# Three small edits to a sequence-block kernel: who issues the first keys' transfer, where a variance row is copied, and how the last product is added and stored

## The reference

```python
# attention, 8 heads of 64: heads 0-3 see the last 32 positions, heads 4-7 every 32nd position
scores = (q @ k.T) / 8; scores = where(mask, scores, -1e9)
x = softmax(scores) @ v                        # heads side by side: 4 x 576 x 512
# gated unit, 512 -> 1024 -> 512
h = gelu(x @ w_in); u, v = h[..., :512], h[..., 512:]
v_n = layer_norm(v) * g_ln
x = x + (u * (w_sg @ v_n + b_sg)) @ w_out      # w_sg mixes the 576 tokens
# norm and feed-forward, 512 -> 2048 -> 512
xn = layer_norm(x) * g_ch                      # over the 512 features
out = x + relu(xn @ w_ch1) @ w_ch2
```

## Time and profile before

| what | value |
|---|---|
| median of 3 runs | 666.21 us (666.0, 666.21, 667.43) |
| profiled execution, its own time | 666.58 us |
| its span | 664.8 us, 14064 instructions |
| PE busy, PE weight loads busy | 655.3 us (99%), 622.8 us (94%) |
| DVE, ACT, POOL busy | 529.1 us (80%), 356.8 us (54%), 245.9 us (37%) |
| chain that ended last | PE 89%, DVE 4%, issue 2%, ACT 2%, POOL 2% |

### The profile page before, as it was taken

How to read it: one execution, slowest core, us unless ns; L and a number is a source line. 1 busy time by engine, 2 the same in 40 slices (tenths; PEclk the granted TensorE clock), 3 DMA queues, 4 the chain that set the end, 5 groups by cost and what they waited for, 6 DMA issues and landing times.

```text
span 664.8 us, 14064 instructions
## 1 busy us (share of the span) xinstructions
PE 655.3 (99%) x5160; PEld 622.8 (94%) x5160; DVE 529.1 (80%) x1162; ACT 356.8 (54%) x897; POOL 245.9 (37%) x258
## 2 busy tenths in 40 slices
PE   8999999999999999999999999999999999999997
PEld 4679998999899998999999999999999999999997
DVE  5967866887679868998876885786999898898883
ACT  6866864488347844434563462345684344444440
POOL 0477240635152438468436447223001412113011
PEclk9999999999999999999999999999999999999999
DMA  8660007000530051128353667869952726517301
GB/s 296 258 241 4 1 3 278 36 1 2 186 146 2 1 176 59 56 69 291 119 171 121 199 241 251 306 216 348 303 171 84 290 72 246 165 58 282 90 19 53
DMA packets 49924, 98.25 MB, mean 148 GB/s; under 512 B 4673, under 2 KB 33217, under 8 KB 47297
## 3 DMA queue, kind: packets, MB, share of 16 engines
q1 hardware_dynamic: 49152, 96.16, 42.2%
q0 software_dynamic: 704, 1.21, 0.8%
HBM read 64.83 MB, written 32.52 MB: 146 GB/s over the span
## 4 chain that ended last, share of the span: by engine, by line
PE 89%; DVE 4%; issue 2%; ACT 2%; POOL 2%; DVEq 0%; POOLq 0%; ACTq 0%
PE pair L1886 17%; PE pair L1888 17%; PE pair L1887 17%; PE pair L1677 9%; PE pair L1679 9%; PE pair L1678 9%; PE pair L1701 3%; PE pair L1734 3%; PE pair L1716 3%; ACT probs L1026 1%; DVE stage L1546 1%; PE pair L1685 1%; DVE res L1406 1%; DVE acc_a L489 1%; PE pair L1797 1%
## 5 line engine op out<-in xcount | busy, mean ns | idle before, releaser
L1886 PE MATMUL pair<-xf_hi,w_hi 128*128 128x288 f32 x896 | 265.6, 296 | 0.2
L1887 PE MATMUL pair<-xf_lo,w_hi 128*128 128x288 f32 x896 | 264.5, 295 | 0.0
L1888 PE MATMUL pair<-xf_hi,w_lo 128*128 128x288 f32 x896 | 263.6, 294 | 0.0
L1888 PEld LDWEIGHTS pair<-xf_hi,w_lo 128*128 128x128 f32 x896 | 168.8, 188 | 0.0
L1886 PEld LDWEIGHTS pair<-xf_hi,w_hi 128*128 128x128 f32 x896 | 167.9, 187 | 0.8 <-ACT rstd L1103 0.7
L1887 PEld LDWEIGHTS pair<-xf_lo,w_hi 128*128 128x128 f32 x896 | 168.2, 188 | 0.0
L1131 ACT ACTIVATE xf_hi<-res 128x576 fp32r<-128x576 f32 x140 | 94.3, 683 | 89.1 <-PE pair L1888 71.9
L1546 DVE TENSOR_TENSOR stage<-pair,stage 128x576 f32<-128x576 f32 x136 | 100.7, 752 | 39.5 <-PE pair L1888 33.3
L567 DVE TENSOR_TENSOR xf_lo<-res,xf_hi 128x576 fp32r<-128x576 f32 x140 | 109.8, 793 | 14.7 <-ACT xf_hi L1131 14.2
L1012 POOL TENSOR_TENSOR xr<-xr,stage 128x576 f32<-128x576 f32 x16 | 32.9, 2058 | 165.7 <-DVE stage L1546 165.6
L1223 ACT ACTIVATE stage<-stage 128x576 f32<-128x576 f32 x64 | 43.6, 683 | 79.8 <-DVE stage L1546 79.7
(11 more groups left out here) (134 smaller groups left out, 1285.0 us busy)
## 6 DMA issues: line engine op xcount, KB each, us to landing
hid_scratch<-stage SPq DMA_DIRECT2D x64, 288.0 KB, 3.5
res<-hid_scratch SPq DMA_DIRECT2D x16, 1152.0 KB, 6.8
w_raw<-w_ff_dram SPq DMA_DIRECT2D x16, 512.0 KB, 4.2
v_sb<-vW_dram SPq DMA_DIRECT2D x16, 384.0 KB, 6.7
xr<-x_scratch SPq DMA_DIRECT2D x16, 288.0 KB, 3.0
out_dram<-xr SPq DMA_DIRECT2D x16, 288.0 KB, 3.3
k_sb<-kT_dram SPq DMA_DIRECT2D x15, 304.0 KB, 6.3
q_sb<-qT_dram SPq DMA_DIRECT2D x15, 288.0 KB, 6.2
```

The costliest lines, as they stand in the source:

```text
L1886: pe.matmul(dst, wh, xh, start=(start and x == 0), stop=False)
L1887: pe.matmul(dst, wh, xl, start=False, stop=False)
L1888: last = pe.matmul(dst, wl, xh, start=False, stop=(stop and x == n - 1))
```

## The change

It has three parts.

First, the first keys' transfer leaves SP's list and becomes the first instruction of ACT's program. On SP the masks' transfer is now second, and everything behind it moves up one place. The warm-up ahead of the first scores has five matmuls and not six.

Second, on ACT, `copy_variance(b - 1, 0)` moves in periods 1 and 2 from the end of t = 0 to just behind the exponentials of step 0.

Third, for the last batch alone, the last product's two halves are handled apart: PE signals `half_ready` when half 0 of its last piece is done, DVE adds half 0 then and half 1 when the product is complete, and SP issues one store of 144 KB for each half in place of one of 288 KB.

```diff
--- before.py
+++ after.py
@@ -77,6 +77,7 @@
 SOLO_WIN_ACT = 2
 WIN_HALVES = (slice(GATE, 2 * GATE), slice(0, GATE))
 EARLY = 4
+NQ_FIRST, NK_FIRST = 2 * QB, 2 * QB + STRIDE
 
 
 FORMS = 7
@@ -351,9 +352,11 @@
         hid_stored = [sem(f"hid_stored{i}") for i in range(4)]
         raw_in = [sem(f"raw_in{i}") for i in range(4)]
         step_ready = sem("step_ready")
+        half_ready, half_added = sem("half_ready"), sem("half_added")
         y_added = sem("y_added")
         waited = sem("waited")
         stored = [sem(f"stored{i}") for i in range(4)]
+        stored_half = sem("stored_half")
 
         block = ctx.enter_context(nc.Block())
 
@@ -632,9 +635,8 @@
                         load_win(0)
                     nq, nk = 0, 0
                     if first and pair == 0:
-                        nq, nk = 2 * QB, 2 * QB + STRIDE
+                        nq, nk = NQ_FIRST, NK_FIRST
                         sp.dma_start(q_sb[:, 0, 0:nq], qT[b, :, 0, 0:nq]).then_inc(q_first, 16)
-                        sp.dma_start(k_sb[:, 0, 0:nk], kT[b, :, 0, 0:nk]).then_inc(k_first, 16)
                         sp.dma_start(mask_raw[:, 0:2 * P], masks[:, 0:2 * P]).then_inc(mask_in, 16)
                     sp.dma_start(q_sb[:, pair, nq:S], qT[b, :, pair, nq:S]).then_inc(q_in[pair], 16)
                     sp.dma_start(k_sb[:, pair, nk:KPAD], kT[b, :, pair, nk:KPAD]).then_inc(k_in[pair], 16)
@@ -726,6 +728,14 @@
                 c, t = divmod(i, 2)
                 sp.dma_start(output_at(i), x_dram[n].rearrange("p (c t) -> p c t", c=KC)[
                     :, 2 * c:2 * c + 2, t * HALF:(t + 1) * HALF]).then_inc(xr_in[i], 16)
+
+            def store_last_half(j):
+                if j == 0:
+                    sp.wait_ge(half_added, 1)
+                else:
+                    sp.wait_ge(drained, (B * LOCKSTEPS + B) * FORMS)
+                c = 2 + j
+                sp.dma_start(out[:, c, (B - 1) * S:(B - 1) * S + HALF], output_at(2)[:, j, :]).then_inc(stored_half, 16)
 
             def store_y(n, i):
                 if i == 2:
@@ -816,11 +826,14 @@
                 store_y(n, 1)
                 if following:
                     load_x(n + 1, 1)
-                store_y(n, 2)
                 if following:
+                    store_y(n, 2)
                     load_x(n + 1, 2)
+            for j in range(2):
+                store_last_half(j)
             for i in range(4):
-                sp.wait_ge(stored[i], 16 * B)
+                sp.wait_ge(stored[i], 16 * (B if i != 2 else B - 1))
+            sp.wait_ge(stored_half, 32)
 
         @block.gpsimd
         def _(pool):
@@ -1173,6 +1186,7 @@
                     if t < QUADS:
                         exps(b + 1, 2 * t)
                     if b >= 1 and t == 0:
+                        copy_variance(b - 1, 0)
                         sum_hi(4 * b - 1)
                     if b >= 1 and t == 1:
                         copy_variance(b - 1, 1)
@@ -1184,8 +1198,6 @@
                         exps(b + 1, 2 * t + 1)
                     if t < NMIX // 2:
                         round_gated(b, 2 * t)
-                    if b >= 1 and t == 0:
-                        copy_variance(b - 1, 0)
 
             def last_period(b):
                 gelus(b, last=True)
@@ -1199,6 +1211,7 @@
                     first_high(g)
                     rest_high(g)
 
+            act.dma_start(k_sb[:, 0, 0:NK_FIRST], kT[0, :, 0, 0:NK_FIRST]).then_inc(k_first, 16)
             for s in range(SOLO_STEPS):
                 if LAG <= s < STEPS:
                     copy_pT(0, s - LAG)
@@ -1565,9 +1578,24 @@
             def c12(m):
                 combine(m, P3, 1, 1)
 
+            def c21_halves(m):
+                dve.wait_ge(half_ready, 1)
+                dve.wait_ge(y_added, 4 * (B - 1) + Y_ADDED[P7])
+                dve.wait_ge(drained, m * FORMS + DRAINED[P3])
+                for j in range(2):
+                    if j == 1:
+                        wait_product(dve, m, P4)
+                    x = output_at(2)[:, j, :]
+                    last = dve.tensor_tensor(x, product_at(m, P4)[:, j, :], x, ALU.add)
+                    if j == 0:
+                        last.then_inc(half_added, 1)
+                last.then_inc(drained, 1)
+
             def c21(m):
                 if m < B * LOCKSTEPS:
                     combine(m, P4, 2, 2)
+                elif m == B * LOCKSTEPS + B - 1:
+                    c21_halves(m)
                 else:
                     combine(m, P4, None, 2)
 
@@ -1851,7 +1879,7 @@
                     group(b, NGELU + NMIX + i)
 
             pe.wait_ge(warm_ready, 1)
-            warm_up(6)
+            warm_up(5)
             for s in range(SOLO_STEPS):
                 if s < TWINS:
                     scores(0, s, first=True)
@@ -1919,6 +1947,8 @@
                 for j in range(2):
                     last = block_product(product_at(m, i)[:, j, :], (2 * p, 2 * p + 1), i, ((0, j), (1, j)), g % FORMS,
                                          p == 0, p == PIECES - 1)
+                    if j == 0 and n == B - 1 and i == P4 and p == PIECES - 1:
+                        last.then_inc(half_ready, 1)
                 last.then_inc(step_ready, 1)
 
             for n in range(B):
```

## The result

The changed kernel takes 666.01 us (median of 22 runs, 664.77 to 667.39) and the kernel before, run beside it, 667.47 us (22 runs, 666.0 to 669.49): a ratio of 0.998, 95% interval 0.9972 to 0.9987. That is 1.46 us between the medians and 1.3 by the ratio, right at the 0.2% that the prediction named as its limit. The forecast was 1.49 us less, but counted from 666.21, the median of three runs, and so at 664.7 with a range up to 665.8: the measured time lies 0.2 us above the range.

What follows compares the result with a forecast made beforehand. PE, busy 655.3 of 664.8 us, was taken as the bound, so only its waits, start and tail could gain. Start 0.29, variance copy 0.49 and tail 0.71 summed to 1.49 us: 664.7 us against 666.21, range 664.0 to 665.8.

Steps and rivals of the forecast that it cites:

- the median of the runs is 666.21, and I state the forecast against that: Whole kernel: the base from which the forecast time of 664.7 us was counted.
- Whatever is gained ahead of 40 us goes through to the end: Start: gains there reach the end, as PE then works back to back and transfers move with it.
- the first term of the sum: Start: five warm-ups instead of six gain 0.29 us, or 0.43 if the clock's rise moves along.
- Rival D: Start: keys landing after 3.54 idle PE, the clock rises later, four slow steps end at 666.7 us; chance 0.06.
- First scores at 3.54: Start: one warm-up less lets the first scores begin at 3.54 instead of 3.97, keys landing 0.4 us earlier.
- The loss of 0.14 us to the clock: Second scores: starting at 6.03, they run 0.37 us at half pace before the clock's rise near 6.4 us.
- All that SP issues behind them comes 0.47 us sooner as well: SP's queue at the start: transfers behind the masks come 0.47 us sooner.
- Rival A: Start: ACT's table load precedes the keys' transfer, scores start at 4.5, 0.5 us later; 665.5 us, chance 0.10.
- The variance copy: Period 2's transposes near 207 us: PE's wait for ACT's copy goes, gaining 0.49 us; nothing in period 1.
- Rival C: Period 2 or both: the 0.33 us on DVE and ACT return as a PE wait; 665.0 to 665.4 us, chance 0.10.
- The tail: Behind the last matmul: 0.31 us from the split addition and 0.4 from the half-size store, 0.71 us together.
- Rival B: Tail: the last store lands no sooner; 665.1 us, chance 0.12.

Runs made afterwards that it cites:

- e5: The changed kernel again, on another chip: median 666.86 us (12 runs), 0.9989 of the kernel before.
- e14: The changed kernel a third time, on a fourth chip: median 666.85 us (11 runs), 0.9992 of the kernel before.
- e6: The changed kernel with six warm-ups, keys still issued by ACT: median 665.96 us (12 runs), 0.998 of the kernel before.
- e7: The changed kernel with the whole first part undone (keys by SP, six warm-ups): median 666.08 us (12 runs), 0.9985 of the kernel before.
- e4: The changed kernel with four filling matmuls in PE's wait near 37 us: median 665.8 us (12 runs), 0.998 of the kernel before.
- e15: The changed kernel with the four filling matmuls, on a fourth chip: median 665.29 us (6 runs), 0.9969 of the kernel before.
- e13: The kernel before with the first part alone, on a fourth chip: median 667.16 us (11 runs), 1.0007 of the kernel before.
- e11: The changed kernel with the last quarter added in two halves but stored by one transfer: 666.04 us (one run).
- e1: The kernel before with the first part alone (keys by ACT, five warm-ups): median 668.29 us (12 runs), 1.0014 of the kernel before.
- e10: The changed kernel with the four filling matmuls, on a third chip: 665.35 us (6 runs), 0.9971 of the kernel before.
- e9: The kernel before with the first part alone plus the four filling matmuls: 666.6 us (12 runs), 0.9992 of the kernel before.
- e8: The kernel before with variance copy and tail parts plus the four filling matmuls: median 665.82 us (12 runs), 0.9982 of the kernel before.
- e16: The kernel before with variance copy and tail parts alone, on a fourth chip: median 666.28 us (11 runs), 0.9988 of the kernel before.
- e2: The kernel before with the earlier variance copy alone: median 667.28 us (12 runs), 1.0002 of the kernel before.
- e3: The kernel before with the split addition and store of the last product alone: median 666.77 us (12 runs), 0.9991 of the kernel before.
- e12: The changed kernel with the first keys issued by SP ahead of the masks, five warm-ups: 667.6 us (one run).

## Why the prediction was right or wrong

**The base was wrong, and that the sum came out was in part luck.** The forecast difference of 1.49 us compares with 1.46 between the medians of the first measurement, but the same pair gave 0.35 and 0.44 us on two other chips (e5, e14). What put the time above the range was the base, "the median of the runs is 666.21, and I state the forecast against that". It was a low draw: three runs from a kernel whose 22 runs have a median of 667.47, 1.26 us more, and 667.1 to 667.3 on four chips more. The page's span of 664.8 was a low one too, with neither a stretch near 38 us nor a pause at 317 or 442. The range allowed for tenths of a microsecond between runs, where one kernel's own runs spread over 3.

**The step of the mechanism that failed** is "Whatever is gained ahead of 40 us goes through to the end", and with it the first term of the sum, 0.29 us. It read PE's wait of 0.93 us near 37 us as a wait and nothing else. In some runs PE comes out of it at 1.2 GHz for 3.4 us and pays 1.6 us. In kernels with five warm-ups 27% of the runs had the mark of that, with six 7%. Twenty per cent of 1.6 us is 0.3, as much as the forecast gain. That agrees with e6 and e7, which lack the gain and are no slower, but it is not the whole account: the runs at full clock don't show the 0.3 us either. Rival D had a related mechanism, a clock that rises later, but put it at 7 us and not at 38, and gave it 0.06.

**The start, step by step.** First scores at 3.54: right, though with 0.2 us of room and not 0.4, as the keys took 2.6 us to land and not 1.9 to 2.4. The loss of 0.14 us to the clock took the rise for fixed. With five warm-ups and the keys on ACT the eight second matmuls took 0.68 (e4, e15) to 1.16 us (e5), anything from none to all of them at 1.2 GHz. Third scores stood ahead of before's 8.47 by 0.53 (e15), 0.46 (e4), 0.40 (e13), 0.38 (e14), 0.32 (e11), 0.31 (e1), 0.14 (e10) and 0.09 (e9), behind it by 0.12 (changed) and 0.05 (e5). That is 0.25 on average; with six warm-ups they stood from 0.11 ahead (e7, e8, e16) to 0.08 behind (e2). The Trainium skill, page "TensorE: Matmul & The Clock Gate", section "What's actually happening", says that the moment of the rise differs from run to run, by 500 ns either way. The traces agree that it differs, and by more: it rose at 4.7 us in e3 and at 7.2 in e12. "All that SP issues behind them comes 0.47 us sooner as well" was right of the issue and says nothing of the landing: the rest of pair 0's keys took 3.3 to 3.9 us with the keys on ACT, and the second scores waited for them (6.17 for 6.03), which the prediction never listed as a user. Before's 2.5 us was at the low end here too: kernels with the old queue took 2.5 to 3.7. Rival A (table load first) was wrong by the first rows of the trace.

**The variance copy**: 0.49 forecast, 0.47 to 0.49 in every profile that has it, none given back. Rival C is out. **The tail**: 0.71 forecast, 0.77 measured, with 0.31 against 0.28 for the addition and 0.40 against 0.49 for the store. Rival B is out.

**What stays open**: why the first part, or its five warm-ups, makes the stretch near 38 us likelier. The late rise at the start and the fall came together three times in three, 30.7 us apart each time, but shifting the pause near 37 us by itself was not tried. Open too is why the times at full clock don't show the start's gain, and whether the change has a hand in the pauses near 317, 442 and 505 us; no cure for these was tried.

## What to carry to other kernels

When a change is worth a thousandth, take the spread of the kernel's own runs before the forecast, and read each part in the profile by the lag of equal instructions, where the variance copy's 0.48 us came out within 0.01 us each time; the interval of a dozen runs here was 1.4 to 1.7 us wide. A part that depends on the clock or on landings needs several profiles: the start's gain went from -0.12 to 0.53 us. A pause of TensorE cost its own length here and sometimes a stretch at 1.2 GHz behind it, so matmuls without use that fill it can be worth their place: the changed kernel with four of them gave 665.8, 665.35 and 665.29 us, 0.998, 0.9971 and 0.9969 of the kernel before. A transfer issued sooner need not land sooner; look up who waits for each one behind it.

## What the runs showed of the hardware that was not expected

The granted clock fell to 0.50 for 3.4 us behind two pauses of PE of 0.28 us and of 0.94 or 0.95, in the three profiles that show it. The mark of it stood in about a quarter of the runs of kernels with five warm-ups (19 of 70), in 7% of those with six (12 of 175), and in none of 48 with the longer pause filled. The moment at which the clock rose at the start lay between 4.7 and 7.2 us, although PE began at 1.30 us each time. A store of 144 KB landed in 1.8 us beside 2.2 for 288 KB. Loads of 192 KB, third to fifth in SP's order, landed 2.4 to 3.9 us after their issue over all profiles.
